# Expert stage with its hidden rows transposed in 32 x 32 blocks on VectorE instead of on TensorE

## What is computed

```python
# B, H, S, D = 4, 8, 768, 64; n_global = 8, n_local = 96
scores = q @ k.T / sqrt(D) + bias(head, distance); keep = global or local band
a = softmax(where(keep, scores, -1e9)); x = (a @ v)            # -> [3072, 512]
# experts: N, D, E, F = 3072, 512, 8, 1024
logits = x @ w_gate; e = argmax(logits); g = softmax(logits)[e]
x = g * (relu(x @ w1[e]) @ w2[e])                               # row by row
# dense: 512 -> 2048 -> 512
h = x @ w_in
g = (a0 + a1*h + a2*h**2 + a3*h**3) / (1 + |b0|*|h| + |b1|*h**2 + 1e-6)
out = g @ w_out
```

## Time and profile before

| | us |
|---|---|
| median of 3 runs | 1191.56 (1191.04 to 1192.66) |
| the profiled execution | 1188.75 |
| its span in the profile | 1187.1 |

### The profile page before, as it was taken

The page is one execution under the profiler, slowest core; times in us unless marked ns, Lnnn a source line. Parts: engine busy times, 40 slices in busy tenths (PEclk is TensorE's granted clock), DMA queues, the critical chain, the costliest instruction groups (busy, mean ns, idle before and its releaser), DMA issues.

```text
span 1187.1 us, 19291 instructions
## 1 busy us (share of the span) xinstructions
PE 1126.0 (95%) x6205; PEld 926.8 (78%) x6206; DVE 701.1 (59%) x1358; ACT 585.4 (49%) x1049; POOL 257.5 (22%) x189
## 2 busy tenths in 40 slices
PE   3999899869999999999998999999999999999996
PEld 2777777748888888888887887888888888888885
DVE  4788788731111111111125996886896896886874
ACT  3777677512222222222234675655655655655652
POOL 1111111144436637627340001000000100100101
PEclk9999999979999999999999999999999999999998
DMA  8987662166557848848563001001001001000000
GB/s 184 306 204 193 185 167 64 47 229 225 168 204 259 271 162 292 284 147 271 182 234 126 1 1 46 27 1 45 27 0 45 27 0 45 27 0 9 27 1 35
DMA packets 138137, 141.46 MB, mean 119 GB/s; under 512 B 100448, under 2 KB 100448, under 8 KB 137056
## 3 DMA queue, kind: packets, MB, share of 16 engines
q0 software_dynamic: 27584, 92.48, 22.3%
q1 hardware_dynamic: 110496, 48.26, 15.3%
HBM read 117.65 MB, written 23.32 MB: 119 GB/s over the span
## 4 chain that ended last, share of the span: by engine, by line
PE 79%; DVE 12%; ACT 3%; issue 3%; DMA 2%; POOL 0%; SPq 0%; POOLq 0%; DVEq 0%; ACTq 0%
PE bank L977 21%; PE bank L979 21%; PE bank L978 21%; PE bank L861 3%; PE bank L824 3%; PE bank L837 2%; PE bank L1008 2%; PE bank L805 2%; DVE poly L1508 1%; PE bank L881 1%; DVE gl L1530 1%; DVE poly L1506 1%; PE bank L972 1%; DMA routed_x<-xt,slot_now 1%; DVE prob L1189 1%
## 5 line engine op out<-in xcount | busy, mean ns | idle before, releaser
L447 POOL TENSOR_TENSOR w_lo<-stage,w_hi 128x2048 fp32r<-128x2048 f32 x32 | 147.4, 4607 | 58.0 <-DMA w_hi<-in_moe_w_dram 26.2
L977 PE MATMUL bank<-w_hi,gh 128*128 128x512 f32 x384 | 151.1, 393 | 2.4 <-DVE gl L1530 2.4
L977 PE MATMUL bank<-x2Th,w_hi 128*128 128x512 f32 x384 | 149.6, 390 | 1.4 <-ACT ybuf L684 0.9
L979 PE MATMUL bank<-w_hi,gl 128*128 128x512 f32 x384 | 150.2, 391 | 0.0
L978 PE MATMUL bank<-w_lo,gh 128*128 128x512 f32 x384 | 150.2, 391 | 0.0
L979 PE MATMUL bank<-x2Th,w_lo 128*128 128x512 f32 x384 | 149.4, 389 | 0.0
L978 PE MATMUL bank<-x2Tl,w_hi 128*128 128x512 f32 x384 | 149.4, 389 | 0.0
L564 POOL DMA_INDIRECT out_dram<-stage,ids x24 | 28.5, 1188 | 523.1 <-ACT stage L764 505.5
L1421 DVE TENSOR_TENSOR hTl<-bank,hTh 128x512 fp32r<-128x512 f32 x62 | 40.0, 686 | 152.2 <-ACT hTh L689 152.2
L1415 DVE TENSOR_TENSOR xTl<-bank,xTh 128x512 fp32r<-128x512 f32 x31 | 21.4, 692 | 158.9 <-ACT xTh L677 158.9
L673 ACT ACTIVATE hbuf<-bank 128x512 f32<-128x512 f32 x62 | 37.1, 599 | 132.8 <-PE bank L979 132.8
(11 more groups left out here) (202 smaller groups left out, 2315.4 us busy)
## 6 DMA issues: line engine op xcount, KB each, us to landing
w_hi<-in_moe_w_dram POOLq DMA_DIRECT2D x32, 1024.0 KB, 6.1
stage<-in_moe_w_dram POOLq DMA_DIRECT2D x32, 1024.0 KB, 8.2
xg<-routed_x SPq DMA_DIRECT2D x31, 256.0 KB, 2.8
routed_y<-ybuf SPq DMA_DIRECT2D x31, 256.0 KB, 5.4
x<-routed_y SPq DMA_DIRECT2D x6, 1056.0 KB, 5.2
kraw<-in_k_dram SPq DMA_DIRECT2D x24, 256.0 KB, 4.2
qraw<-in_q_dram SPq DMA_DIRECT2D x24, 256.0 KB, 4.5
vraw<-in_v_dram SPq DMA_DIRECT2D x24, 256.0 KB, 4.1
```

Of the source, the lines that this page charges most:

```text
L447: pool.tensor_tensor(w_lo[:, at:at + CH], stage[:, c % 2, :], w_hi[:, at:at + CH].bitcast(F32), ALU.subtract).then_inc(chunk_ready, 1)
L977: pe.matmul(dst, lhs_hi, rhs_hi, start=first, stop=False)
L979: return pe.matmul(dst, lhs_lo, rhs_hi, start=False, stop=last)
```

## The change

- In the expert stage, tiles 0 to 29, `moe_turn_h` is gone from TensorE. VectorE's new `turn_h(t, k)` transposes `hbuf` in blocks of 32 x 32: 8 instructions for each k, one for each pair of a group of 32 rows q and a block column r, each with 8 blocks of 32 x 32 (32 partitions x 256 elements), from `hbuf` into PSUM, where `HB_ps[k]` is the same bank as `HT_ps[k]` was, seen as [128, 8, 64]. `moe_ht` on ScalarE and VectorE then splits by token columns (64 k to 64 k + 64) rather than by blocks of h. The last tile keeps the transposes on TensorE (`last_turn_h`, `last_ht`).
- VectorE's step is `turn_h(t, 0); moe_x(t + 1); turn_h(t, 1); moe_ht(t)`; `turn_h` waits for both halves of the rectified rows (`h_sb`).
- ScalarE's rectification waits for `h_turned` of the tile before; TensorE's up waits in each half for `h_sb` of the tile before.
- `weight_set` takes the number of the expert whose half it overwrites: `up_free` waits on `h_ps` until that expert's last up is done, before the two casts of `w1`; `down_free` waits on `tile_done`, as `half_free` did, behind the first subtraction and before the casts of `w2`. `end_i` has a second row of counts for it, one more VectorE operation.
- On SyncE, ScalarE, TensorE and VectorE the branch is `If(banded > 0)` with the banded path, `Else` the full path.
- The last pair of the last group is done in two halves of 512 elements from `hidden` to `g_low`; `up` signals after each half, and `down` waits for the second half before its fourth matmul.

```diff
-            with pe.If(banded(pe) < 1):
+            with pe.If(banded(pe) > 0):
+                pe_steps()
+            with pe.Else():
                 with pe.Fori(0, B) as b:
                     pe_full(b)
-            with pe.Else():
-                pe_steps()
...
             def moe_up(t, off, e):
                 for n in range(2):
+                    if not isinstance(t, int) or t > 0:
+                        pe.wait_ge(h_sb, 2 * t + n - 1)
...
                 moe_down(t - 1, off_down, e_down)
-                moe_turn_h(t)
                 moe_up(t + 1, off_up, e)
...
+            def turn_h(t, k):
+                if not isinstance(t, int) and k == 0:
+                    dve.wait_ge(ht_lo, 2 * t)
+                dve.wait_ge(h_sb, 2 * t + 2)
+                for q in (2 * k, 2 * k + 1):
+                    for r in range(4):
+                        rows = hbuf[q * QD:(q + 1) * QD, :].rearrange("p (j r i) -> p j r i", r=4, i=QD)[:, :, r, :]
+                        ins = dve.transpose(HB_ps[k][r * QD:(r + 1) * QD, :, q % 2 * QD:(q % 2 + 1) * QD], rows)
+                ins.then_inc(h_turned, 1)
             def moe_ht(t):
+                for k in range(2):
+                    cols = slice(64 * k, 64 * k + 64)
+                    dve.wait_ge(ht_hi, 2 * t + k + 1)
+                    dve.tensor_tensor(hTl[:, :, cols], HB_ps[k], hTh[:, :, cols].bitcast(F32),
+                                      ALU.subtract).then_inc(ht_lo, 1)
...
-            with dve.Fori(0, MT - 1) as t:
-                moe_x(t + 1); moe_ht(t)
+            turn_h(0, 0); moe_x(1); turn_h(0, 1); moe_ht(0)
+            with dve.Fori(1, MT - 1) as t:
+                turn_h(t, 0); moe_x(t + 1); turn_h(t, 1); moe_ht(t)
...
-            def moe_h(t):
+            def moe_h(t, first=False):
                 for n in range(2):
                     act.wait_ge(h_ps, 2 * t + n + 1)
+                    if n == 0 and not first:
+                        act.wait_ge(h_turned, 2 * t)
...
+            def weight_set(s, par, srcs, kinds, next_srcs, next_kinds, old=None):
+                if old is not None:
+                    up_free(old)
                 cast_in(0, par, srcs, kinds)
                 cast_in(1, par, srcs, kinds)
                 for c in range(4):
                     split(s, c, par)
+                    if c == 0 and old is not None:
+                        down_free(old)
...
+                    if last and p == PAIRS - 1:
+                        denominator(g, p, 0)
+                        g_low(g, p - 1)
+                        numerator(g, p, 0)
+                        refine(g, p, 0)
+                        quotient(g, p, 0)
+                        denominator(g, p, 1)
+                        numerator(g, p, 1)
+                        refine(g, p, 1)
+                        quotient(g, p, 1)
+                        g_low(g, p, 0)
+                        g_low(g, p, 1)
+                        continue
```

More of the change, by code:

```diff
@@ L97, in build_program @@
         dest_i = keep("dest_i", [P, MT], I32)
-        end_i = keep("end_i", [P, E], I32)
+        end_i = keep("end_i", [P, 2, E], I32)
         coef = keep("coef", [P, 8])
@@ L186, in build_program @@
         HT_ps = bank[2:4]
+        HB_ps = [bank[2 + k].rearrange("p (j n) -> p j n", j=FB) for k in range(2)]
         Y_ps = bank[4]
@@ L748, in g_high @@
-            def g_high(g, p):
-                r, n = p % 2, g * PAIRS + p
+                act.activation(rec[r][:, k, :], rec[r][:, k, :], ACT.Exp, scale=-1.0).then_inc(rec_ready, 1)
+            def g_high(g, p, half=None):
+                r, n, k = at(g, p, half)
                 act.wait_ge(g_full, n + 1)
@@ L767, in group @@
                 for p in range(PAIRS):
-                    turning = p == PAIRS - 1 and not last
+                    if last and p == PAIRS - 1:
+                        hidden(g, p, 0)
+                        g_high(g, p - 1)
+                        linear(g, p, 0)
+                        recip(g, p, 0)
+                        hidden(g, p, 1)
+                        linear(g, p, 1)
+                        recip(g, p, 1)
+                        g_high(g, p, 0)
+                        g_high(g, p, 1)
+                        continue
                     hidden(g, p)
@@ L1065, in up, with down @@
                                    j == 0, j == KB - 1)
+                    if halves and i == 0:
+                        mm.then_inc(h2_ps, 1)
                 mm.then_inc(h2_ps, 1)
-            def down(g, p, again):
+            def down(g, p, again, halves=False):
                 n = g * PAIRS + p
@@ L1082, in down @@
                         at = SET + f * DM
+                        if halves and (i, j) == (1, 0):
+                            pe.wait_ge(g_lo, n + 2)
                         mm = three(O2_ps[j][:, :], gh[:, p % 2, i, j * P:(j + 1) * P], gl[:, p % 2, i, j * P:(j + 1) * P],
@@ L1094, in group @@
                         down(g - 1, PAIRS - 2, again)
-                    up(g, p)
+                    up(g, p, last and p == PAIRS - 1)
                     if p == 0 and again:
@@ L1111, in _ @@
             down(NG - 1, PAIRS - 2, True)
-            down(NG - 1, PAIRS - 1, True)
+            down(NG - 1, PAIRS - 1, True, True)
         @block.vector
@@ L1361, in dve_full @@
                 assert done[0] == FULL_STEPS
-            with dve.If(banded(dve) < 1):
+            with dve.If(banded(dve) > 0):
+                dve_steps()
+            with dve.Else():
                 dve.wait_ge(tables_in, TI)
@@ L1376, in _ @@
                     low_part(n // 4, n % 4)
-            with dve.Else():
-                dve_steps()
             done[0] = 0
```

153 lines of the change are left out of this document (83 added, 70 removed).

## The result

| | before | changed |
|---|---|---|
| median, us | 1192.11 (1191.04 to 1192.90, 4 runs) | 1165.36 (1164.37 to 1167.43, 4 runs) |
| the profiled execution, us | 1188.75 | 1167.43 |
| its span, us | 1187.1 | 1165.5 |

The ratio is 0.9778 (95%: 0.9761 to 0.9795), 26.5 us less by the ratio; the medians lie 26.8 apart. The two spans differ by 21.6 us only: the profiled execution of before was 2.8 to 3.4 under its median, that of the changed kernel 2.1 over its own. Where these 5 us lie is the second thing that the traces show; the terms come first.

What follows compares the result with a forecast made beforehand. TensorE, busy 95% of the span, was taken as the bound. Terms -25.5 + 3.2 + 2.0 + 1.9 + 1.0 - 4.5 - 4.0 sum to -25.9 us, from a median of 1191.56 to 1165.7 us; range 1160 to 1177.

Steps and rivals of the forecast that it cites:

- Transposes off TensorE: Expert stage, 29 steady tiles: each tile 0.88 us shorter without TensorE's eight transposes, -25.5 us if VectorE and ScalarE keep up.
- d: Time per VectorE block transpose of 32 partitions by 256 elements in the expert stage, taken as 0.45 us (0.33 to 0.69).
- both deadlines: Steady tile: VectorE readies x's low part before up (0.5 us in hand), then the second low part before down (1.3).
- First tiles: Up for tile 1 waits for x's low part behind eight transposes, +3.2 us; half clock behind the wait, +2.0 us.
- Into the dense stage: Before x2's first turn: TensorE waits for VectorE's gate chain, +1.9 us; half of a clock drop entered, +1.0 us.
- Banded path first: Kernel start: VectorE's 4.57 us between branch and first table operation goes and the gain passes on, -4.5 us (0 to -4.6).
- the term for the stage's end: End of attention: the 4.6 us jump over the full path fits in VectorE's 6.0 us of waiting, 0.
- Last pair in halves: End of the dense stage: no wait and no clock drop at the last down, -4.0 us (-1.5 if it slips).
- Release: Expert weights freed in two steps: earlier release adds slack, shorter tiles eat a little of it, 0 us.
- d was never near 0.60: Rivals on slow block transposes: at 0.69 us each, 1225 us, even from 0.60 (7%); at 0.52 to 0.60, 1180 us (11%).
- the jump was saved: Rival on the branch order: the 4.57 us at the start come back in part or whole, 1170 us, 15%.
- the last pair followed: Rival at the end: two engines hand each half back and forth, 1.0 to 4.0 us of gain missing, 1168.5 us, 6%.

## Why the prediction was right, and where not

The forecast was 1165.7 us, the median is 1165.36. By its steps:

- **Transposes off TensorE, -25.5.** Right: 0.89 us a tile. d was 0.47 for 0.45; both deadlines held, the first with 0.66 us in hand, and it is the one that binds. The choice of the chained row of 248 elements over the 0.33 and the 0.69 was what the rest hung on.
- **First tiles, +3.2 and +2.0.** Right: +3.23, and ten matmuls at 0.43, +2.0. Putting tile 0 back on TensorE gave 5.2 us in the profile, 3.1 to 4.9 in the medians and ratios.
- **Into the dense stage, +1.9 and +1.0.** The wait was right (1.88). The half drop came as nothing in this profile. Seven profiles have a wait of 1.87 to 1.89 us there: in six the clock stayed at 1.00 behind it, in one (first tile on TensorE) it fell. After 2.16 us there (two transposes more) it was 0.66 over 4 us, after 2.66 (transposes cut in two) 0.63; after 2.08 us at the end it fell in the earlier trace rows and in the three others with the last pair whole. Half was too much for 1.9 us: one in seven.
- **Left out: the store of y, +0.9.** I wrote that "what follows there on VectorE and ScalarE is tied to TensorE's turn and moves with it". ScalarE's last copy of y hangs on a DMA as well. The wait was 0.75 and 0.93 us with the old tiles and 0.8 to 2.2 with the short ones, so part of the 0.9 is this one execution. Why the store takes longer in some is open.
- **Banded path first, -4.5.** The start was right to 0.04 us. The step that failed is the term for the stage's end, "A 4.6 us jump fits in that 6.0 us: 0". What it says of VectorE held: the row table came about 3 us later, counted from the last slots, and VectorE still waited 4.58 us for xTh behind it. What it left out is the other way from the last slots to the first tile: GpSimd's scatter, SyncE's load, TensorE's turn of x. `row_i` is not on it. With the banded path first, the load even came before the table was done in four of nine profiles (the branches alone: load at 243.36, `row_i` at 243.82). From the last slots to the first turn of x it is 10.2 to 12.2 us in these nine, 11.4 on average, and 9.6 to 10.0 in the three with the full path first, 9.8 on average. So the new order costs some 1.5 us there, and the part should bring 3 us; it brought 4.1 (2.6 to 5.6) alone. The 1.1 between them is within the interval. Why the scatters land later is open. One thing goes with it in all twelve profiles: from 232 to 244 us the queues marked "instruction" in the DMA view carry seven packets (six in one) with the banded path first, one or two with the full path first.
- **Last pair in halves, -4.0.** Right: 4.05 in the profile, 3.8 to 5.0 in the medians.
- **Release, 0.** Right, and the run that undid it shows why.

The rivals: d was never near 0.60; the jump was saved in most part; the last pair followed. That the total came within half a microsecond is luck: the 1.5 and the 0.9 that I missed stand against the 1.0 of a drop that did not come, and the 26.5 us are themselves known only to about 2 (24.4 to 28.5). That the profile of before lay under its median I carried over as a constant 2.81 us. That was right by its size. The likely reason, which only the later profiles suggest, is that its attention stage was the only one of the twelve with no drop of the clock; no second profile of that kernel exists to show it.

The Trainium skill (VectorE: DVE Perf Modes, Rules for kernel authors) sends a 128 x 128 transpose to TensorE where PSUM can take it. This trace disagrees for this kernel: 0.79 us on the engine that bounds it were dearer than 7.5 us on one that rested. It is right where the transposes stand in the chain: for tile 0, going back to TensorE brought 5.2 us in the profile.

## What to carry to other kernels

Work may move to an engine ten times slower at it if that engine rests, but each queue position must be costed by the next thing queued behind it and by who reads that, in the steady loop and apart from it in the first and the last pass, where nothing hides it. When you say that a delay is covered, follow every way that leads through the place, with the DMA queues, and not only the engine whose wait is longest; and check in the program what each reader waits for, since two rows that end together (the row table at 244.72, the load at 244.76) need not depend on each other. Before a single profile is taken as the base, compare its granted clock with that of others: here the way from VectorE's first table operation to the last slots took 225.1 us in the profile of before and 226.4 to 231.3 in the eleven others.

## What the runs showed of the hardware

- A block transpose of 32 partitions x 256 fp32 elements from SBUF into PSUM takes 456 ns, one of 128 elements 301 ns; both start behind an output to other partitions only when the one before has ended, 0.47 us apart for the large ones. Cutting one in two costs 0.06 us, since only 0.1 us overlaps.
- Leaving a branch with a long block behind it costs TensorE 3.4 to 4.3 us with nothing to wait for, much as entering one had cost VectorE 4.57 us. That this is the fetching of code is suggested, not proved: in the DMA view of 4 to 13 us the queues marked "instruction" carry four packets in the three profiles with the full path first and none in the nine others, and at the stage's end it is the other way round, one or two against six or seven.
- TensorE's granted clock falls to half for a few microseconds in the attention stage in eleven of twelve profiles. TensorE is busy some 90% of the stage. In both profiles of the changed kernel the drops between 76 and 192 us come within 3 us behind a stop of 0.98 us, which at other times has no drop behind it.
